# Loads issued one scheduling beat later in a fused attention and two-layer MLP kernel

## The reference

```python
scores = scale * np.matmul(q, k.transpose(0, 1, 3, 2))
thresh = np.max(scores, axis=-1, keepdims=True) - tau
scores = np.where(scores >= thresh, scores, -1000000000.0)
scores = scores - np.max(scores, axis=-1, keepdims=True)
attn = np.exp(scores)
attn = attn / (np.sum(attn, axis=-1, keepdims=True) + 1e-09)
attn_out = np.matmul(attn, v)
# x: (2304, 512)
h = np.maximum(x @ w_in, 0.0);  x = (s * (h * h) + b) @ w_out
h = x @ w_in2;  out = (h * (1.0 / (1.0 + np.exp(-1.702 * h)))) @ w_out2
```

## Time and profile before

| | |
|---|---|
| timed runs | 1027.64, 1029.03, 1027.82 us; median 1027.82 |
| profiled execution, its own time | 1027.64 us |
| its span in the profile | 1025.8 us (1.84 us lie around it) |
| TensorE busy | 990.8 us of the span |
| VectorE, ScalarE, GpSimd busy | 804.2, 601.7, 654.1 us |
| q loads | 48 of 192 KB |
| k loads | 32 of 288 KB |
| mean granted TensorE clock | 0.995 of full speed |

### The profile page before, as it was taken

How to read it: one execution, slowest core, us unless ns; L and a number is a source line. 1 busy time by engine, 2 the same in 40 slices (tenths; PEclk the granted TensorE clock), 3 DMA queues, 4 the chain that set the end, 5 groups by cost and what they waited for, 6 DMA issues and landing times.

```text
span 1025.8 us, 17824 instructions
## 1 busy us (share of the span) xinstructions
PE 990.8 (97%) x5752; PEld 888.2 (87%) x5752; DVE 804.2 (78%) x1753; ACT 601.7 (59%) x1100; POOL 654.1 (64%) x708
## 2 busy tenths in 40 slices
PE   5878999999999999999999999999999999999998
PEld 4667888888888888888899999889898999989897
DVE  7899999999999999999546765877666776656573
ACT  6766666666666666665555755654545545454453
POOL 5648997778888788886657775544534445444442
PEclk9999999999999999999999999999999999999999
DMA  6128977798887888778833541022123221231212
GB/s 206 57 76 205 230 203 207 193 246 224 203 216 191 222 211 216 211 179 219 204 103 127 167 165 46 24 80 82 42 83 110 75 83 42 82 123 63 82 46 79
DMA packets 100843, 144.24 MB, mean 141 GB/s; under 512 B 10640, under 2 KB 72208, under 8 KB 100752
## 3 DMA queue, kind: packets, MB, share of 16 engines
q1 hardware_dynamic: 100752, 143.11, 50.0%
HBM read 102.96 MB, written 4.72 MB: 105 GB/s over the span
## 4 chain that ended last, share of the span: by engine, by line
PE 84%; DVE 10%; issue 2%; DMA 2%; ACT 1%; POOL 0%; SPq 0%; DVEq 0%; ACTq 0%
PE shared L791 12%; PE y_ps L810 11%; PE y_ps L908 9%; PE shared L884 9%; PE scores L908 9%; PE scores L710 7%; PE scores L884 7%; PE scores L767 6%; PE scores L791 5%; PE y_ps L830 4%; DVE scores L992 3%; DVE prob L1018 3%; PE scores L830 1%; DVE blocks L1032 1%; PE shared L767 1%
## 5 line engine op out<-in xcount | busy, mean ns | idle before, releaser
L1211 ACT ACTIVATE prob<-scores,neg_max 128x576 f32<-128x576 f32 (+1 forms) x160 | 118.6, 741 | 136.8 <-DVE scores L992 131.1
L1539 POOL TENSOR_TENSOR a_sum_lo<-a_sum,a_hi 128x256 fp32r<-128x256 f32 x96 | 70.0, 740 | 187.8 <-DVE scores L1114 124.7
L1495 POOL TENSOR_TENSOR w_lo<-w_raw,win_hi 128x512 fp32r<-128x512 f32 x96 | 129.0, 1343 | 23.2 <-ACT win_hi L1247 19.5
L992 DVE TENSOR_SCALAR_CACHE_REDUCE scores<-scores,consts 128x576 f32<-128x576 f32 (+1 forms) x160 | 129.2, 807 | 17.1 <-PE scores L710 16.3
L1502 POOL TENSOR_TENSOR w_lo<-w_raw,wout_hi 128x512 fp32r<-128x512 f32 x96 | 125.7, 1310 | 25.6 <-ACT wout_hi L1254 25.6
L1489 POOL TENSOR_SCALAR prob<-prob,row_inv 128x576 f32<-128x576 f32 (+1 forms) x160 | 125.1, 794 | 24.3 <-DVE row_inv L1006 24.2
L1018 DVE SCALAR_TENSOR_TENSOR prob<-scores,limit,prob 128x576 f32<-128x576 f32 (+1 forms) x160 | 128.4, 808 | 0.6 <-ACT prob L1211 0.3
L1032 DVE STREAM_TRANSPOSE blocks<-prob 128x576 f32<-128x576 f32 (+1 forms) x136 | 97.1, 750 | 1.2 <-DMA prob_t<-blocks 0.7
L791 PE MATMUL shared<-act_hi,win_hi 128*128 128x384 f32 x276 | 93.6, 339 | 3.5 <-POOL w_lo L1495 1.9
L710 PE MATMUL scores<-k_hi,q_hl 128*128 128x288 f32 (+1 forms) x320 | 78.4, 327 | 18.9 <-DVE prob L1018 12.4
L1055 DVE SCALAR_TENSOR_TENSOR g_lo<-gate,consts,g_hi 128x384 fp32r<-128x384 f32 x96 | 94.1, 981 | 0.0
(11 more groups left out here) (154 smaller groups left out, 2931.6 us busy)
## 6 DMA issues: line engine op xcount, KB each, us to landing
w_raw<-slabs SPq DMA_DIRECT2D x93, 512.0 KB, 4.0
a_raw<-twin_in SPq DMA_DIRECT2D x24, 512.0 KB, 4.6
o_raw<-twin_out SPq DMA_DIRECT2D x24, 512.0 KB, 3.6
prob_t<-blocks SPq DMA_DIRECT2D x96, 120.0 KB, 3.3
k_raw<-k SPq DMA_DIRECT2D x32, 288.0 KB, 4.9
q_raw<-q SPq DMA_DIRECT2D x48, 192.0 KB, 4.5
prob_t<-blocks SPq DMA_DIRECT2D x96, 96.0 KB, 3.4
v_sb<-v SPq DMA_DIRECT2D x26, 320.0 KB, 4.8
```

Source lines behind the costliest of these rows:

```text
L992: nc.vector.tensor_scalar(place, place, scale_c[0:m, :], None, ALU.mult, ALU.min, accum_out=neg_max[0:m, j % STATS:j % STATS + 1]).then_in ...
L1211: nc.scalar.activation(prob[0:m, j % PROBS, :].rearrange("p (a n) -> p a n", a=2), scores[j % 2][0:m, :, 0:HALF], ACT.Exp, bias=neg_max[0: ...
L1495: nc.gpsimd.tensor_tensor(in_of(w_lo, n), in_of(w_raw, n), win_hi[n % IN_HI][:].bitcast(F32), ALU.subtract).then_inc(win_lo_ready, 1)
```

## The change

Loads move in SP's loop, and four key splits move one beat.

- `q_load_beat` goes. Query loads are issued one beat before the split instead of two. 44 of the 45 loads in the loop move one beat later (the first stays in beat 0).
- `key_load_beat` goes. A key whose slot is free in the beat before its split is loaded at the head of that beat: 22 of the 30 keys in the loop move one beat later, keys 2, 3, 8 and 9 stay.
- The `+ 1` after `key_free_beat(e)` in `key_split_beat` goes. That moves the split of keys 16, 17, 30 and 31 one beat earlier on ScalarE and GpSimd. Their loads are issued one beat earlier too, by a second loop that stands after the weights and queries and ahead of the values of the beat.
- The default of `key_free_beat` for a slot with no earlier key becomes 0 instead of -1.

```diff
-def q_load_beat(i):
-    return max(0, q_split_beat(i) - 2)
...
 def key_free_beat(e):
-    return key_tiles(key_before(e))[-1] // 2 + 1 if key_before(e) is not None else -1
+    return key_tiles(key_before(e))[-1] // 2 + 1 if key_before(e) is not None else 0
...
-    return max(FIRST_BEAT[TILE_AT[key_tiles(e)[0]][0]] - 4 + e % 2, key_free_beat(e) + 1, e % 2)
-
-
-def key_load_beat(e):
-    return max(0, key_free_beat(e), key_split_beat(e) - 2)
+    return max(FIRST_BEAT[TILE_AT[key_tiles(e)[0]][0]] - 4 + e % 2, key_free_beat(e), e % 2)
...
             for beat in range(BEATS):
                 for e in range(2, HEADS):
-                    if key_load_beat(e) == beat:
+                    if max(0, key_split_beat(e) - 1) == beat and key_free_beat(e) <= beat:
                         load_k(e)
...
                 for i in range(3, len(Q_LOADS)):
-                    if q_load_beat(i) == beat:
+                    if max(0, q_split_beat(i) - 1) == beat:
                         load_q(i)
                 if beat == 1:
                     for n in range(IN_LEAD + 1):
                         load_weights(n)
+                for e in range(2, HEADS):
+                    if key_split_beat(e) - 1 == beat and key_free_beat(e) > beat:
+                        load_k(e)
```

## The result

The changed kernel is slower: median 1037.19 us of five runs (1033.08 to 1042.41), before 1028.45, also of five. The ratio is 1.0073, with a 95% interval of 1.0043 to 1.0102, so about 7.5 us are lost. The profiled execution of the changed kernel has a span of 1036.7 us, 10.9 more than the one before. One execution of one kernel further down took 1101.46 us at a mean granted clock of 0.85, where all others have 0.99 or more; its time enters no ratio.

The account below looks back on a forecast made before the run. TensorE, busy 329.80 of 330 us in the beats, was taken as the bound; all terms were 0 except load 39's 0.7 to 1.1 us, taken as 0.8, giving 1028.6 us, range 1027.0 to 1032.5.

Parts of the forecast that it names:

- Faster: Rival: shorter TensorE holes ahead of 110 us and one clock dip gone, 2.0 + 0.6 us gained, 1025.2 us; chance 0.07.
- Late queries and their places: Beats: late split_q delays gate_of, gated, hidden; load 39 costs 0.7 to 1.1 us, loads 30, 42, 24, 45 nothing.
- the 1.7 us that I took as its cover: Before a short beat: slack from gate_of to gated (1.10) and gated to hidden (0.71), 1.81 us together, taken as 1.7.
- The landing: Moved query loads land as loads at the same places before, 4.2 to 5.0 us; load 39 is 2.4 us late.
- my upper bound: All moved query loads landing in 6.2 us, with SP's 0.44 us: 8.4 us lost.
- My slower rival: Query loads join runs of moves and everything there lands later, 5.5 us: about 3.5 us lost, 1031.3 us; chance 0.36.
- My sign for it: Query loads' median landing passing 5.1 us would show the forecast wrong; the slower rival decides above 0.2% from about there.
- SP's queue: Runs of moves in batches 2 and 3: one more issue makes what follows 0.44 us later; load 39 costs 1.1, not 0.7.
- The moved blocks: Perhaps 0.4 us later; VectorE's turn waits for them at one place, covered by 2.66 us before a long beat.
- Keys and the start: Later keys and early splits of 16, 17, 30, 31 cost 0; start costs 0, with 0.3 us to either side.
- the time ahead of 110 us moves by more than 0.5 us: Sign at the kernel's start: a shift above 0.5 us there would show the forecast wrong.
- The estimate for one DMA: GpSimd-path fit, 2.0 us plus bytes over 436 GB/s: 2.5 us for 192 KB, load 39 in time, sum 0.

Follow-up runs that it names:

- query-only kernel: Against the kernel before, only the query loads go one beat later; keys load and split as before. Ratio 1.0050, median 1035.06 us.
- spare loads of 8 KB: Changed kernel, queries loaded two beats ahead, plus a 16-column copy of each query from 12 on, fetched at the later place into an unread buffer. Ratio 1.0024.
- second six queries early: Changed kernel with query loads 30, 33, 36, 39, 42 and 45 (second of each run of moves) back in their old beat. Ratio 1.0046, repeated 1.0045.

## Why the prediction was wrong

**What bounds the kernel, and the sign.** Right: nothing to win in the beats, TensorE as the clock of everything, and a loss only through waits that get through to it. Faster had 0.07 and fell. The forecast itself, 0.8 us lost, was wrong by a factor of nine, and the range (to 1032.5) did not hold the 1037.19.

**Late queries and their places.** Right in kind, and partly in place. I named splits 39, 45, 24 and 30 as the longest at 1.5 to 3 us; 30, 36, 39, 42 and 45 had 2.5 to 3.8, and 24 had none. The path `split_q`, `gate_of`, `gated`, `hidden` and the 1.7 us that I took as its cover ahead of a short beat came out exactly. ScalarE's waits of 2.69, 2.54, 2.59 and 3.79 us left holes of 0.98, 0.88, 0.92 and 2.09 us on TensorE, so 1.66 to 1.71 us were covered each time. Load 45, with 3.8 us of cover, left none. What was wrong is how late the queries were.

**The landing, the step that failed first.** I read each new place's landing from the load that stood there before, 4.2 to 5.0 us, and said of the run that its bytes were the same in all. They are not the same within the run: a query of 192 KB came in from the idle time ahead of it, and keys changed their places. The landing at the place of 280.77 went from 5.0 to 7.7 us, above even the 6.2 of my upper bound. For loads 36 and 39 it was 6.7 us, where the places had 4.2 and 4.9. The query-only kernel puts a share to it: 9.6 us of waits for queries without the keys' move, 16.7 with it. My slower rival had the mechanism word for word (landings lengthen together) and a price of 3.5 us, half of what was measured. My sign for it, a median landing over 5.1 us, did not fire: the median of all query loads stayed at 4.5 us, since the few loads at the end of the runs don't move it.

**SP's queue, mis-sized in the same sum.** I took 0.44 us for one issue more. For load 42 it was 2.1 us, and with 0.8 us of landing that made the longest wait and the largest hole. Part of it is chance, since the long issue of 1.83 us need not fall there in another execution.

**The moved blocks, the step that failed second.** I gave them 0.44 us, SP's issue of one more load, and looked only at VectorE's transposes, which a long beat covers. That left out that they are DMAs too, behind the same bytes, and that TensorE's own context matmuls wait for them. The cover there could have been read before: the last of the eight moves, issued at 272.33, landed 3.6 us later at 275.9, and the context matmuls started at 278.57. These rows are of the kernel before.

```profile
DMA to landing us min/median/max: 3.6/3.6/3.6
```

```profile
278.57 0.55 PE L767 MATMUL scores<-prob_t,v_sb 128*64 128x192 f32 x4
```

So 2.7 us there; worked out the same way for the five other runs it is 1.5, 2.2, 2.3, 1.0 and 0.8 us, against an extra landing of the last move of 3.3 us in the first run and 2.4 in the third. TensorE's two holes for moved blocks, of 0.44 and 0.83 us, are in just these two. With the second queries in time the kernel still loses 0.45%, through this path (TensorE's context waits 3.9 us).

**Keys and the start.** Right within what can be told: keys 1.0009, the early splits nothing that can be seen. The sign "the time ahead of 110 us moves by more than 0.5 us" fired in the profile after (2.0 us) without being the change's, so it was a bad sign: the start varies by more than that between executions. Of the others, ScalarE waited at 8 splits where I had a dozen, VectorE's wait in `gated` grew by 5.6 us (2 to 5), and TensorE's named waits for `gate` were three, of 3.9 us together, where I had one or two, of about 1.

**The estimate for one DMA.** The estimate of 2.5 us for 192 KB by the Trainium skill (DMA: Bandwidth & Descriptors, Anatomy of one DMA) is a third of what the load in the run took. The page gives the fit for each DMA. Here what counts is what stands in the queue ahead of it.

## What to carry to other kernels

A load that moves to another place in a shared queue changes the landing of everything behind it, so price its bytes and its issue for each transfer behind it in the same burst, not only its own lateness. For each of those transfers work out the cover at its own consumer before calling it free: here the moved blocks, which the prediction waved through, cost some 0.45% with most late queries out of the way, and the late queries 0.26% with no block late. And a load's lead is not counted in beats but in what stands ahead of it; issued ahead of the burst, in the time when SP waits anyway, one beat was as good as two (ratio 0.9998).

## What the runs showed of the hardware

- Loads of one size from one queue landed after 2.3 us (192 KB with little around it, the least of the earlier trace rows) and after 7.7 us (the last of a burst). The landing followed what stood ahead and not the load's own size: the spare loads of 8 KB landed after 3.4 to 7.6 us.
- A load that nothing in the beats waits for cost up to 0.64% (with 6.9 MB more in 36 loads; 0.09% of it goes with the keys), through the transfers behind it.
- Cutting that load to 8 KB with the same number of issues took away more than half of its cost.
- SP took about 0.6 us to issue one move and 0.33 to 0.45 us for most loads of keys and queries, and 12 moves in the profile before (11 after) took over 1 us. Eight moves took 5.1 to 6.4 us, nearly a whole beat of 6.5.
- The start of the kernel differs between executions. The changed kernel and the one with the second six queries early are the same program up to beat 44. From 10 to 100 us the granted clock was 0.92 in the profile of one and 0.94 in that of the other, and TensorE began beat 20 later than in the kernel before by 2.0 us and 0.5 us. Single runs of the kernel before took from 1026.0 to 1034.1 us, so that differences under some 0.15% could not be told here with a dozen runs.
